# Angle weights before the second chunk, the first angles before the second scores, an early sine, a later wait: retention, token mixer and MLP on one core

## The chip, the cores and the metric

The kernel runs on one core of a Trainium2 chip. The time is device microseconds of one execution, as a median of several. Engines are named as the profile names them: PE is TensorE (PEld its weight loads), DVE is VectorE, ACT is ScalarE, POOL is GpSimd, SP is SyncE; a trailing q, as in SPq, is an engine's sequencer, which also issues DMAs.

## What is computed

Three layers in float32, on 2 batches, 768 tokens and 512 channels (8 heads of 64):

```python
# 1. retention, per head: decayed state, scaled readout
for t in range(S):
    state = gamma * state + outer(k[t], v[t])
    y[t] = scale * (q[t] @ state)
# 2. angles, token mixer, channel layer (x = y with the heads side by side)
theta = x @ w_theta
u = x + w_tok_r @ (x * cos(theta)) + w_tok_i @ (x * sin(theta))
x = u + relu(u @ w_ch)
# 3. MLPs over tokens and over channels
u = x + (relu(x.T @ w_tok1) @ w_tok2).T
out = u + relu(u @ w_ch1) @ w_ch2
```

## The kernel before, in words

**Products.** Most products are done as three reduced-precision matmuls on split operands (helper `three`, L778): each operand is a high part (rounded, written by ACT) plus a low part (the rest, written by DVE or POOL). So every weight and every activation is split before PE can use it. Semaphores order everything; each engine runs its own instruction list strictly in the order written.

**Head of the kernel.** The tokens go through in 12 chunks of 128, numbered g (6 per batch). For a chunk PE runs `scores(g)` (keys times queries, L788), `keys_values(g)` (the chunk's part of the state, L802), `outputs(g)` (L817: first the part read from the state, L827, then the part from the weighed scores, L837), `turn_x` (a transpose, L843) and `theta(g)` (the angles, L854: 12 matmuls that accumulate over 4 channel blocks; for g = 0 the first six wait for the first half of the split angle weights, the other six for the second half). DVE runs `weigh(g)` (L592, scores times the causal decay; it needs `scores(g)`, and `outputs(g)` and `scores(g + 1)` need it), `advance_state` (L597), `finish_x` (L609, it needs `outputs`), `x_low` (L616), and for g = 0 the two `theta_low` (L575), the low halves of the angle weights. ACT runs `x_high` (L473) and for g = 0 the two `theta_high` (L457), later the sine and the cosine of the angles (`waves`, L488). POOL runs `decay_keys(g)` (L377, needs chunk g in memory; it is written one chunk ahead) and `carry_state` (L388).

**Loads.** SP issues in this order: queries and keys of chunk 0 (0.5 MB), its other half (0.5 MB), the output decay (0.25 MB), chunk 1 (1 MB), the two halves of the angle weights (0.5 MB each, into `raw`), chunk 2, a third of a token weight, and then one chunk and one third at a time. Chunk 3 and later wait until `outputs` of the chunk three before has freed the buffer. ACT issues the small constants.

**Order of PE at the start (L882 to L905).** Two dummy matmul calls on a zeroed tile (`keep_warm`), `scores(0)`, `outputs(0)`, `keys_values(0)`, `scores(1)`, `keys_values(1)`, `outputs(1)`, `theta(0)`, `scores(2)`, `keys_values(2)`, `outputs(2)`, `scores(3)`, `turn_x(0)`, `theta(1)`, and from there one such round per chunk.

**Order of DVE at the start (L689 to L714).** `weigh(0)`, `advance_state(0)`, `finish_x(0)`, `weigh(1)`, `x_low(0)`, `theta_low` twice, `advance_state(1)`, `finish_x(1)`, `weigh(2)`, `x_low(1)`, and so on.

**The token mixer** is a two-by-two block scheme of 7 products of 4 steps each (28 steps, `mix`, L865). DVE adds each result into `res` (`keep_y`, L663; semaphore `y_kept`). The last two products write PSUM banks 0 to 3. ACT and POOL split `res` into `ut` (`ut_high`, `ut_low`) for the next layer, the first token half while the mixer still runs.

**The channel layer** (`channels(q)`, L906, 16 steps) writes banks 4 and 5 in turn. Its first step waits for all 28 `y_kept`. `turn_x2(n)` (L921) writes banks 6, 7 and 0 and comes after several channel steps. The MLPs follow.

Of the kernel before, what the change touches and what calls it, by code (L numbers as in the profile page):

```python
# [7 lines left out]
ACT = mybir.ActivationFunctionType  # L8

P = 128  # L10
# [3 lines left out]
NG = B * NC  # L14
# [42 lines left out]
STEPS = PRODUCTS * NPAIR  # L57
# [33 lines left out]
def retention_mixer_mlp(nc, qkv, theta_w, tok, weights, consts, out):  # L91
    with ExitStack() as ctx:
        def sb(name, shape, dt=F32, within=ctx):
            return within.enter_context(nc.sbuf_tensor(name, shape, dt))

        def sem(name):
            return ctx.enter_context(nc.semaphore(name))

        cst = sb("cst", [P, N_CONST])

        res = sb("res", [P, B, NK, S])

# [5 lines left out]
        with ExitStack() as first:  # L108
            idle = sb("idle", [P, DM], within=first)
# [59 lines left out]
        def f32(ap):  # L169
            return ap.bitcast(F32)  # L170
# [23 lines left out]
        def turned(n):  # L194

            return n // 3 % B, n // 6 * 3 + n % 3
# [4 lines left out]
        def tokens(tile, k):  # L201

            return res[:, tile, k, 0:DM] if tile < B else res[:, :, k, DM:S]
# [33 lines left out]
        idle_ready = sem("idle_ready")  # L237
# [25 lines left out]
        y_kept = sem("y_kept")  # L263
# [20 lines left out]
        def split_done(eng, i):  # L284
            if i < MIDDLE:
                eng.wait_ge(middle_lo, i + 1)
            else:
                eng.wait_ge(late_lo, i - MIDDLE + 1)
# [35 lines left out]
        @block.sync  # L324
        def _(sp):
            def load_chunk(g):
                if g >= NQ:
                    sp.wait_ge(y_ready, g - NQ + 1)
                if g == NQ:
                    sp.wait_ge(kv_ready, 1)  # L330
                sp.dma_start(qkv_in[:, g % NQ, :], qkv[g]).then_inc(chunk_in[g % NQ], 16)

            def load_piece(i):
                if i >= NSTAGE:
                    split_done(sp, i - NSTAGE)
                sp.dma_start(stage[:, i % NSTAGE, :], weights[i]).then_inc(piece_in[i % NSTAGE], 16)

            def load_third(e):

                q, at = (2, 1, 0)[1 + e // 3], slice(e % 3 * THIRD, (e % 3 + 1) * THIRD)  # L340
                if e == 3:
                    sp.wait_ge(theta_lo, 2)
                sp.dma_start(raw[:, q, at], tok[2 * q, :, at]).then_inc(third_in[e], 16)

            sp.dma_start(qkv_in[:, 0, 0:2 * DM], qkv[0, :, 0:2 * DM]).then_inc(first_qk_in, 16)
            sp.dma_start(qkv_in[:, 0, 2 * DM:4 * DM], qkv[0, :, 2 * DM:4 * DM]).then_inc(chunk_in[0], 16)
            sp.dma_start(cst[:, C_OUT:N_CONST], consts[:, C_OUT:N_CONST]).then_inc(decay_in, 16)
            load_chunk(1)
            for i in range(2):
                at = slice(i * THETA_HALF, (i + 1) * THETA_HALF)  # L350
                sp.dma_start(raw[:, 0, at], theta_w[:, at]).then_inc(theta_in[i], 16)
            for g in range(2, NG):
                load_chunk(g)
                if g < 8:
                    load_third(g - 2)

            sp.wait_ge(zr_ready, NG)
            sp.wait_ge(zi_ready, NG)
            for i in range(N_PIECES):
                load_piece(i)  # L360
            for tile in range(TILES):
                for n in range(NK):
                    sp.wait_ge(sum_kept, tile * NK + n + 1)
                    to = out[tile, n, :, 0:DM] if tile < B else out[:, n, :, DM:S].rearrange("b p t -> p b t")
                    sp.dma_start(to, tokens(tile, n)).then_inc(out_sent, 16)
            sp.wait_ge(out_sent, 16 * TILES * NK)
# [89 lines left out]
        def _(act):  # L456
# [52 lines left out]
                act.activation(u_half(0, b, k, half), res_half(b, k, half), ACT.Copy).then_inc(ut_hi, 1)  # L509

            act.dma_start(cst[:, 0:C_OUT], consts[:, 0:C_OUT]).then_inc(const_in, 16)
            act.wait_ge(const_in, 16)
            for g in range(NG + 2):
                if g < NG:
# [59 lines left out]
        def _(dve):  # L574
            def theta_low(i):  # L575
                at = slice(i * THETA_HALF, (i + 1) * THETA_HALF)
                dve.wait_ge(theta_hi, i + 1)
                dve.scalar_tensor_tensor(out=w_sq[:, 1, at], in0=raw[:, 0, at], scalar=TURNS, in1=f32(w_sq[:, 0, at]),  # L578
                                         op0=ALU.mult, op1=ALU.subtract).then_inc(theta_lo, 1)
# [12 lines left out]
            def weigh(g):  # L592
                dve.wait_ge(score_ready, g + 1)
                dve.tensor_tensor(prob[:, :, :], ps[:, BK_SCORE:BK_SCORE + 2, :], causal[:, :, :],  # L594
                                  ALU.mult).then_inc(prob_ready, 1)

            def advance_state(g):  # L597
                b, c = g // NC, g % NC
                if c == NC - 1:
                    return  # L600
                dve.wait_ge(kv_ready, b * (NC - 1) + c + 1)
                new, kv = state[:, (g + 1) % 2, :], ps[:, BK_STATE, 0:H * D // 2]
                if c == 0:
                    dve.tensor_scalar(new, kv, 1.0, None, ALU.mult).then_inc(state_ready, 1)
                else:
                    dve.wait_ge(carried_ready, b * (NC - 2) + c)
                    dve.tensor_tensor(new, kv, carried[:, :], ALU.add).then_inc(state_ready, 1)
# [13 lines left out]
            def reduce_angle(g):  # L621
                t = turn[:, g % 2, :]
                dve.wait_ge(whole_ready, g + 1)
                if g >= 2:
                    dve.wait_ge(zi_ready, g - 1)

                dve.scalar_tensor_tensor(out=t, in0=fold[:, g % 2, :], scalar=-ROUND, in1=bank(BK_THETA + g % 2),
                                         op0=ALU.add, op1=ALU.subtract).then_inc(frac_ready, 1)
                dve.wait_ge(frac_ready, g + 1)
                dve.tensor_scalar(t, t, 0.5, -0.5, ALU.min, ALU.max).then_inc(angle_ready, 1)  # L630
# [65 lines left out]
            for g in range(NG + 2):  # L696
                if 0 <= g - 2:
                    reduce_angle(g - 2)
                if g < NG:
                    advance_state(g)  # L700
                    finish_x(g)
                if g + 1 < NG:
                    weigh(g + 1)
                if g < NG:
                    x_low(g)
                if g == 0:
                    for i in range(2):
                        theta_low(i)
                if g >= NG - 1:
                    z_low(g - (NG - 1))  # L710
                if g >= 2:
                    turn_parts(g - 2)
                    if g < 8:
                        token_low(1 - (g - 2) // 3, (g - 2) % 3)  # L714
# [62 lines left out]
        def _(pe):  # L777
# [107 lines left out]
            for g in range(NG):  # L885
                if g and g % NC < NC - 1:
                    keys_values(g)
                outputs(g)
                if g == 0:
                    keys_values(0)  # L890
                if g == 1:
                    theta(0)
                if g + 1 < NG:
                    scores(g + 1)
                if g >= 2:
                    turn_x(g - 2)
                    theta(g - 1)
# [8 lines left out]
            def channels(q):  # L906
                half, b, n = q // (B * NK), q // NK % B, q % NK
                if q == 0:
                    split_done(pe, P_T12 - 1)
                    pe.wait_ge(y_kept, STEPS)  # L910
                if q >= 2:
                    pe.wait_ge(x2_kept, q - 1)
                for k in range(NK):
                    if n == 0:
                        pe.wait_ge(ut_lo, half * B * NK + b * NK + k + 1)
                    mm = three(ps[:, BK_M + q % 2, 0:HS],
                               lambda l: w_sq[:, l, k * DM + n * P:k * DM + (n + 1) * P],
                               lambda r: u_half(r, b, k, half), k == 0, k == NK - 1)
                mm.then_inc(m_ready, 1)

            def turn_x2(n):  # L921
                b, c = turned(n)
                pe.wait_ge(x2_kept, (n // 3 + 1) * NK)
                if n >= 3:
                    pe.wait_ge(x2_lo, n - 2)
                for k in range(NK):
                    mm = pe.transpose(ps[:, BK_X2[n % 3], k * P:(k + 1) * P],  # L927
                                      res[:, b, k, c * P:(c + 1) * P], ident)
                mm.then_inc(x2_ready, 1)
# [141 lines left out]
```

## Time and profile before

| | |
|---|---|
| median of 3 runs | 449.81 us (449.34 to 450.46) |
| profiled execution | 449.38 us, span 447.6 us |
| PE busy | 437.8 us, 98% of the span |
| DVE, ACT, POOL busy | 210.4, 127.9, 99.1 us |
| moved by DMA | 38.29 MB, mean 86 GB/s |

The span runs from the first to the last instruction; the rest of the execution's time lies around it. Busy time says how long an engine worked, not that it set the time. The chain of waits is followed back from the last instruction to whatever released each step. What sets the time at a place is read from that chain and from the idle time in front of an instruction.

### The profile page before, as it was taken

How to read it: one execution, taken by the hardware profiler on the slowest of the kernel's cores; microseconds unless marked ns; L12 is line 12 of the kernel's file. 1: busy time of each engine (PE TensorE's matmuls, PEld its weight loads, DVE VectorE, ACT ScalarE, POOL GpSimd, SP SyncE). 2: the span in 40 equal slices, each digit the busy share in tenths (PEclk: the TensorE clock that was granted, in tenths of full speed). 3: DMA queues.
4: the chain of work that ended last, by engine and by line, in shares of the span. 5: the costliest groups of instructions: out<-in, count | busy, mean ns of one | idle time of the engine just before them, and what ended most of it. 6: DMA issues, size and time to landing. Idle time of an engine off the chain costs nothing.

```text
span 447.6 us, 6232 instructions
## 1 busy us (share of the span) xinstructions
PE 437.8 (98%) x2676; PEld 382.3 (85%) x2676; DVE 210.4 (47%) x304; ACT 127.9 (29%) x194; POOL 99.1 (22%) x80
## 2 busy tenths in 40 slices
PE   7799999999999999999999999999999999999996
PEld 4587878899999999999889888888888888888885
DVE  3789998799999993244335211112211113111113
ACT  0455654734455456012313211111111110111110
POOL 2422241000200009940998940000000000000000
PEclk9999999999999999999999999999999999999999
DMA  8955697540784111030241000000200001000002
GB/s 309 395 218 202 267 235 168 105 142 0 183 182 154 47 49 48 13 129 1 94 142 47 1 0 1 0 0 12 84 1 0 0 1 73 21 1 0 1 0 94
DMA packets 9980, 38.29 MB, mean 86 GB/s; under 512 B 993, under 2 KB 2145, under 8 KB 8161
## 3 DMA queue, kind: packets, MB, share of 16 engines
q1 hardware_dynamic: 7856, 28.31, 17.3%
q0 software_dynamic: 1952, 9.44, 9.2%
q8 instruction: 21, 0.34, 0.3%
q10 hardware_dynamic: 144, 0.14, 0.1%
q14 instruction: 7, 0.05, 0.0%
HBM read 34.75 MB, written 3.15 MB: 85 GB/s over the span
## 4 chain that ended last, share of the span: by engine, by line
PE 95%; DVE 2%; DMA 1%; ACT 1%; issue 0%; DVEq 0%; ACTq 0%
PE ps L780 85%; PE ps L797 3%; PE ps L837 3%; PE ps L851 2%; PE ps L927 1%; PE ps L811 1%; PE ps L827 1%; DMA qkv_in<-qkv 1%; DVE w_sq L578 1%; DVE res L774 1%; DVE prob L594 1%; ACT L477 0%; ACT w_sq L460 0%; ACT x_hi L477 0%; DVE res L613 0%
## 5 line engine op out<-in xcount | busy, mean ns | idle before, releaser
L780 PE MATMUL ps<-u,w_a 128*128 128x512 f32 x432 | 103.3, 389 | 0.0
L768 DVE SCALAR_TENSOR_TENSOR w_sq<-ps,w_sq 128x512 fp32r<-128x512 f32 x36 | 24.9, 692 | 156.7 <-ACT w_sq L561 156.7
L780 PEld LDWEIGHTS ps<-u,w_a 128*128 128x128 f32 x432 | 81.1, 188 | 16.8
L780 PE MATMUL ps<-tw,zs 128*128 128x384 f32 x504 | 88.1, 334 | 0.0
L780 PEld LDWEIGHTS ps<-tw,zs 128*128 128x128 f32 x504 | 87.3, 188 | 0.1
L561 ACT ACTIVATE w_sq<-ps 128x512 fp32r<-128x512 f32 x36 | 21.6, 599 | 168.0 <-PE ps L780 168.0
L780 PE MATMUL ps<-w_sq,ch_a 128*128 128x512 f32 x216 | 51.9, 389 | 0.0
L780 PE MATMUL ps<-w_sq,w_b 128*128 128x512 f32 x216 | 51.4, 389 | 0.0
L780 PEld LDWEIGHTS ps<-w_sq,w_b 128*128 128x128 f32 x216 | 40.5, 188 | 8.4
L780 PEld LDWEIGHTS ps<-w_sq,ch_a 128*128 128x128 f32 x216 | 40.5, 188 | 8.4
L780 PE MATMUL ps<-ut,w_sq 128*128 128x384 f32 x192 | 35.6, 339 | 0.7 <-issue 0.7
L504 ACT ACTIVATE zs<-z 128x768 fp32r<-128x768 f32 x28 | 23.7, 846 | 37.0 <-PE ps L780 37.0
L780 PEld LDWEIGHTS ps<-ut,w_sq 128*128 128x128 f32 x192 | 32.9, 188 | 1.0 <-issue 1.0
L780 PE MATMUL ps<-w_sq,x_hi 128*128 128x512 f32 x96 | 30.8, 402 | 2.3 <-DVE w_sq L578 2.3
L400 POOL TENSOR_TENSOR ut<-res,ut 128x384 fp32r<-128x384 f32 x16 | 16.6, 1068 | 33.0 <-ACT ut L509 33.0
L780 PEld LDWEIGHTS ps<-w_sq,x_hi 128*128 128x128 f32 x96 | 17.1, 188 | 5.9 <-issue 2.2
L584 DVE TENSOR_TENSOR tw<-raw,tw 128x768 fp32r<-128x768 f32 x21 | 20.8, 988 | 0.0
L780 PE MATMUL ps<-w_sq,x_lo 128*128 128x512 f32 x48 | 18.8, 392 | 0.0
L385 POOL TENSOR_TENSOR k_dec<-qkv_in,cst 128x512 f32<-128x512 f32 x10 | 11.5, 1148 | 30.7 <-DMA qkv_in<-qkv 26.8
L731 DVE SCALAR_TENSOR_TENSOR res<-ps,res 128x384 f32<-128x384 f32 x16 | 8.9, 558 | 19.3 <-PE ps L780 19.3
L467 ACT ACTIVATE tw<-raw 128x768 fp32r<-128x768 f32 x21 | 17.4, 830 | 1.0 <-DMA raw<-tok 1.0
L780 PE MATMUL ps<-u,w_b 128*128 128x512 f32 x72 | 17.4, 395 | 0.0
(83 smaller groups left out, 473.1 us busy)
## 6 DMA issues: line engine op xcount, KB each, us to landing
qkv_in<-qkv SPq DMA_DIRECT2D x11, 1024.0 KB, 6.1
stage<-weights SPq DMA_DIRECT2D x17, 512.0 KB, 3.3
raw<-tok POOLq DMA_DIRECT2D x7, 1152.0 KB, 8.9
cols_out<-res SPq DMA_DIRECT2D x12, 256.0 KB, 2.1
raw<-tok SPq DMA_DIRECT2D x6, 384.0 KB, 8.1
raw<-tok POOLq DMA_DIRECT2D x3, 384.0 KB, 9.2
qkv_in<-qkv SPq DMA_DIRECT2D x2, 512.0 KB, 5.0
raw<-theta_w SPq DMA_DIRECT2D x2, 512.0 KB, 8.6
```

The lines of the kernel that those rows point to most:

```text
L385: pool.tensor_tensor(heads(k_dec[:, n % 2, :]), heads(qkv_in[:, g % NQ, 2 * DM:3 * DM]), key_decay, ALU.mult).then_inc(key_ready, 1)
L400: pool.tensor_tensor(u_half(1, b, k, half), res_half(b, k, half), f32(u_half(0, b, k, half)), ALU.subtract).then_inc(ut_lo, 1)
L467: act.activation(tw[:, p % 2, 0, at], raw[:, W_RAW[p], at], ACT.Copy).then_inc(tok_hi, 1)
L504: act.activation(zs[:, s % NZ, 0, :], z[:, Z_KIND[p], i, :], ACT.Copy, scale=Z_SIGN[p]).then_inc(z_hi, 1)
L561: act.activation(h2[:, f % 2, 0, :], bank(BK_H2 + f % 4), ACT.Relu).then_inc(h2_hi, 1)
L584: dve.tensor_tensor(tw[:, p % 2, 1, at], raw[:, W_RAW[p], at], f32(tw[:, p % 2, 0, at]), ALU.subtract).then_inc(tok_lo, 1)
L731: dve.scalar_tensor_tensor(out=part, in0=ps[:, BK_M + q % 2, 0:HS], scalar=0.0, in1=part, op0=ALU.max, op1=ALU.add).then_inc(x2_kept, 1)
L768: dve.scalar_tensor_tensor(out=h2[:, f % 2, 1, :], in0=bank(BK_H2 + f % 4), scalar=0.0, in1=f32(h2[:, f % 2, 0, :]), op0=ALU.max, op1=ALU. ...
L780: mm = pe.matmul(dst, left(l), right(r), start=first and n == 0, stop=last and n == 2, skip_group_check=True)
L797: mm = pe.matmul(ps[:, BK_SCORE + r, i * P:(i + 1) * P], qkv_in[rows, g % NQ, DM + i * P:DM + (i + 1) * P], qkv_in[rows, g % NQ, i * P:(i ...
L837: mm = pe.matmul(ps[cols, BK_Y + r, i // 2 * P:(i // 2 + 1) * P], qkv_in[:, g % NQ, 3 * DM + h * D:3 * DM + (h + 1) * D], prob[:, r, i * P ...
L851: mm = pe.transpose(ps[:, BK_XROW, k * P:(k + 1) * P], res[:, b, k, c * P:(c + 1) * P], ident)
```

## The change

The two loads of the angle weights move ahead of the load of chunk 1. PE runs `theta(0)` right after `keys_values(0)`, ahead of `scores(1)`. DVE runs `weigh(1)` after `x_low(0)` and the two `theta_low`. ACT gets one extra sine of one column at its start, ahead of its wait for the constants; it reads the zeroed tile and nothing reads its result. In the channel layer the wait for all 28 `y_kept` moves from the first channel step to the first `turn_x2`.

```diff
@@ sync @@
-            load_chunk(1)
             for i in range(2):
                 at = slice(i * THETA_HALF, (i + 1) * THETA_HALF)
                 sp.dma_start(raw[:, 0, at], theta_w[:, at]).then_inc(theta_in[i], 16)
+            load_chunk(1)
@@ scalar @@
             act.dma_start(cst[:, 0:C_OUT], consts[:, 0:C_OUT]).then_inc(const_in, 16)
+
+            act.wait_ge(idle_ready, 1)
+            act.activation(spare[:, :], idle[:, 0:1], ACT.Sin)
             act.wait_ge(const_in, 16)
@@ vector @@
-                if g + 1 < NG:
+                if 0 < g < NG - 1:
                     weigh(g + 1)
                 if g < NG:
                     x_low(g)
                 if g == 0:
                     for i in range(2):
                         theta_low(i)
+                    weigh(1)
@@ tensor @@
                 outputs(g)
                 if g == 0:
                     keys_values(0)
-                if g == 1:
                     theta(0)
                 if g + 1 < NG:
                     scores(g + 1)
@@ channels @@
                 if q == 0:
                     split_done(pe, P_T12 - 1)
-                    pe.wait_ge(y_kept, STEPS)
@@ turn_x2 @@
                 pe.wait_ge(x2_kept, (n // 3 + 1) * NK)
+                if n == 0:
+                    pe.wait_ge(y_kept, STEPS)
```

## Rows read from the trace of the kernel before

**Rows 1.** The page: busy time, share and instructions of each engine; the granted clock.

```profile
PE 437.8 (98%) x2676; PEld 382.3 (85%) x2676; DVE 210.4 (47%) x304; ACT 127.9 (29%) x194; POOL 99.1 (22%) x80
...
PEclk9999999999999999999999999999999999999999
```

**Rows 2.** Chain that ended last, in order of time: start us, us, what.

```profile
5.36 2.10 PE ps L797 x16
...
9.94 0.49 PE ps L811 x16
...
10.95 0.61 DVE res L613
...
11.63 1.28 ACT L477
...
12.92 0.63 ACT x_hi L477
13.55 0.96 ACT w_sq L460
...
17.80 1.65 PE ps L780 x6
19.45 1.12 PE ps L797 x16
...
20.59 1.24 DVE prob L594
...
21.87 1.09 PE ps L837 x16
...
24.64 2.75 PE ps L780 x12
27.40 0.62 PE ps L811 x16
28.01 0.60 PE ps L827 x16
```

**Rows 3.** Timeline of PE at the first angles: start us, us, line, [idle before <-releaser].

```profile
15.91 0.70 PE L780 MATMUL ps<-w_sq,x_hi 128*128 128x512 f32 x2 [1.99 <-DVE w_sq L578]
```

**Rows 4.** Timeline of DVE and POOL around the split of the angle weights.

```profile
14.53 1.23 DVE L578 SCALAR_TENSOR_TENSOR w_sq<-raw,w_sq 128x1024 fp32r<-128x1024 f32 x1 [0.26 <-ACT w_sq L460]
...
15.68 2.07 DVE L578 SCALAR_TENSOR_TENSOR w_sq<-raw,w_sq 128x1024 fp32r<-128x1024 f32 x1
...
9.81 1.04 POOL L385 TENSOR_TENSOR k_dec<-qkv_in,cst 128x512 f32<-128x512 f32 x1 [2.05 <-DMA qkv_in<-qkv]
14.86 1.80 POOL L385 TENSOR_TENSOR k_dec<-qkv_in,cst 128x512 f32<-128x512 f32 x1 [4.01 <-DMA qkv_in<-qkv]
```

**Rows 5.** Timeline of SP, then the last line of the view of L351.

```profile
2.81 0.97 SPq L351 DMA_DIRECT2D raw<-theta_w  x2
...
DMA to landing us min/median/max: 8.2/8.6/9.0
```

**Rows 6.** Groups by line: every table load of ACT.

```profile
L477 ACT ACT_TABLE_LOAD x1 | 1.3, 1283 | 11.6 <-DVE res L613 11.6
L494 ACT ACT_TABLE_LOAD x1 | 1.3, 1283 | 0.0
```

**Rows 7.** Timeline of PE's first work; scores (L797) at 6.3 us, then chunks 0 to 3.

```profile
1.46 3.78 PE L786 MATMUL ps<-idle 128*128 128x512 f32 x4 [1.46 <-DVE idle L689]
...
L797 PE MATMUL ps<-qkv_in x6: 417/418/418, 6.0 to 6.4; 64*128 64x128 f32 x6
...
L797 PE MATMUL ps<-qkv_in x64: 272/272/579, 5.4 to 23.8; 64*128 64x128 f32 x64
```

**Rows 8.** Timeline, 170 to 180 us: the end of the mixer, the channel layer's start.

```profile
168.46 11.74 POOL L400 TENSOR_TENSOR ut<-res,ut 128x384 fp32r<-128x384 f32 x11 [33.02 <-ACT ut L509]
...
175.47 0.56 DVE L687 TENSOR_TENSOR res<-res,ps 128x384 f32<-128x384 f32 x1 [2.57 <-PE ps L780]
...
176.13 4.05 PE L780 MATMUL ps<-ut,w_sq 128*128 128x384 f32 x22 [0.69 <-issue]
```

More of the change, by code:

```diff
@@ L99, in retention_mixer_mlp @@
         cst = sb("cst", [P, N_CONST])
+        spare = sb("spare", [P, 1])
         res = sb("res", [P, B, NK, S])
```

## The prediction

> **What bounds the kernel now.** I read the page first. PE is busy for 98% of the span and nothing else comes near [rows 1], so an edit can pay or cost only where PE stands still or where the order of its work changes. The chain of waits says where: from 21.87 us on it holds PE alone, apart from one hole of 0.69 us at the channel layer (below) and the last additions into the result. Before 21.87 us it hops between engines [rows 2]. So I worked out the head of the kernel step by step up to `outputs(2)`, which starts its second part at 21.87 us, and took the rest as PE work that shifts with it. The rounds that follow cannot soak up a shift, since each engine's list there is unchanged and PE never waits.
>
> In the head the reader is to see two chains. One leads to the angles: `finish_x(0)` ends at 10.95 + 0.61 = 11.56, a table load of 1.28, `x_high` 0.63, the first `theta_high` 0.96, then `theta_low` twice on DVE, and PE's last six angle matmuls 17.80 + 1.65 = 19.45 [rows 2]. PE waits for it: 1.99 us ahead of the first angle matmul [rows 3], while it has already done `scores(1)` and `outputs(1)` in the time before. The other is the loop scores, `weigh`, `outputs`: scores 1.12, `weigh` 1.24, small gaps; from 19.45 to 21.87 that is 2.42 us, during which PE has `keys_values` and the state part of `outputs` (0.62 + 0.60) to do beside `weigh` [rows 2].
>
> **The table load.** The extra sine puts a table load near 1.5 us, where ACT has nothing to do until 11.56. Will the later ones go? The trace has two: one before the first copy, one before the first sine, and none after it, though copies, absolute values and ReLUs follow [rows 6]. So the set that holds the sine holds the rest, and both loads go from their places. The second was on ACT alone. The first is in the chain: 1.28 us. `x_high(0)` then runs 11.63 to 12.26, the first `theta_high` to 13.22, and `theta_low` could start at 13.24 instead of 14.53. The Trainium skill (ScalarE: Activation LUTs, What ACT_TABLE_LOAD costs) gives about 2.7 us for a load; the row says 1.28. By the page the gain would be 1.4 us more.
>
> **The loads.** The second half of the angle weights was issued at about 3.3 us and took 9.0, so it landed at 12.3; the first landed at 2.81 + 8.2 = 11.0 [rows 5]. ACT would want them at 12.26 and 13.22. Earlier loads therefore gain nothing by themselves. But chunk 1 trades places with them: the same bytes stand ahead of it as stood ahead of the second half, so it lands near 12.3. Behind it is `decay_keys(1)` on POOL, which ran at 9.81 and took 1.04 [rows 4]; now it starts at about 12.3 to 13.0, in the middle of DVE's splitting.
>
> **What POOL then costs.** The trace shows such a meeting. `decay_keys(2)` started at 14.86, when chunk 2 landed, and took 1.80 instead of 1.04, with the first `theta_low` (14.53 to 15.76, 1.23 us) beside it; the second `theta_low` took 2.07 instead of 1.23 [rows 4]. The extra times fit an order of turns: POOL waits for the first, the second waits for POOL; the second ended 17.75 - 15.76 = 1.99 after the first. After the change there are two such meetings. `x_low(0)` and `decay_keys(1)` end at about 14.0 together (12.3 + 0.69 + 1.04, in either order, give or take 0.1). The first `theta_low` goes from 14.0 to 15.2. `decay_keys(2)` still comes at 14.86 (the bytes ahead of chunk 2 are the same), so the second `theta_low` ends at 15.2 + 1.99 = 17.2. PE's second six follow: 17.25 + 1.65 = 18.9. Of the 1.28 us of the table load only 19.45 - 18.9 = 0.55 is left.
>
> **The order of PE.** Before, `scores(1)`, `weigh(1)` and `outputs(1)` ran in the shadow of the angle chain. Now they stand behind `theta(0)`, and nothing of PE's can fill the shadow: from 9.94 + 0.49 = 10.43 to about 15.3 PE is idle. After the angles come scores and `weigh` (2.42), the second part of `outputs(1)` (1.09), and again scores and `weigh` (2.42): 5.93 us, so that `outputs(2)` starts its second part at 18.9 + 5.93 = 24.8 instead of 21.87. Head: +2.9 us. `keys_values(1)` and the state part of `outputs(1)` stay beside `weigh(1)`, at a gap of 0.1 at most. `weigh(1)` moved on DVE delays nobody: DVE is free at 17.2 and the scores come at 20.0. Chunk 4 waits for `outputs(1)` and is issued 8 us later (near 22 instead of 13.96), but `scores(4)` is needed only after `theta(1)`, beyond 28.01 + 2.9, and 9 us from issue to landing is the longest of rows 5; if it came 1 us late, that would add 1 us, which I leave to the range.
>
> **The channel layer.** The last `mix` ends about 175.4; DVE's last `keep_y` runs 175.47 to 176.03; `channels(0)` starts at 176.13 after 0.69 us of idle [rows 8]. Its data is the first token half, all of it split long before: POOL begins that half at 168.46 and needs about 1.07 each for 8, done at 172. Its bank was last read two products earlier. So the hole closes: -0.69 us, at worst 0. Where the wait went, at the first `turn_x2`, it is over some 12 us before PE arrives.
>
> **The sum.** +2.9 - 0.7 = +2.2 to +2.3 us. Against the profiled execution's own 449.38 us (span 447.6) this gives 451.6; that run lies 0.43 below the median of 449.81, so the median to expect is 452.1, +0.5%. About 0.3% is what a measurement of this kernel can tell from no change, so 448.5 to 451.2 counts as the same.
>
> **Rival 1: PE's clock falls in the new pause.** The granted clock in the page reads 9 in every slice [rows 1], yet the durations show two levels: a score matmul takes 418 ns at 6.3 us and 272 ns later, and the 16 of `scores(0)` took 2.10 us against 1.12 [rows 2, 7], so PE ran at 1.2 GHz for its first 5.6 us of work (from 1.46 to past 7.0) and then at 2.4 GHz. The pauses that it withstood here are at most 2 us; the new one is 4.9. If PE comes back at the lower level for as long as at the start, until about 20.9, the first six angle matmuls (2.75 / 2 warm) take 2.8 and end at 18.1, the second six take 3.3 in place of 1.65, and end at 21.4 instead of 18.9: +2.5, and part of the next scores up to +1.0. With +3.0 the median is 455.1. For it: the pause is more than twice any that the trace has. Against it: no row shows a fall after work has begun. If it comes but lifts again by 18 us, it costs only 0.2 and my forecast stands. The Trainium skill (TensorE: Matmul & The Clock Gate, HAM oscillation) warns that pauses between bursts of matmuls bring the half-rate clock back; by it this rival would be the forecast. Chance 0.27.
>
> **Rival 2, on the other side: POOL and DVE do not meet.** If chunk 1 lands so early that `decay_keys(1)` is over by 12.3 (landing before 11.2), the first `theta_low` starts at 13.24. Without the second meeting either, both end at 13.24 + 2 x 1.23 = 15.7, the angles at 17.4, `outputs(2)` at 23.3: head +1.45, sum +0.8, 450.6, no measurable change. With the second meeting alone: 13.24 + 3.22 (as from 14.53 to 17.75) + 1.70 = 18.2, sum +1.5, 451.4. It decides for "the same" once the angles end before 18.0. Against it: the queue's order. Chance 0.18. To be faster by over 0.3% the angles would have to end before 15.3, which two `theta_low` alone rule out on these rows; I keep 0.05 for what they don't show.
>
> **Rival 3: the edits don't do what they say.** The table load stays in its place (+1.3) or the hole at the channel layer stays (+0.7): 452.8 to 453.4. Against it rows 6 and 8. Chance 0.05.
>
> **How the numbers follow.** The forecast has 0.45: 452.1, its own range 451.3 to 453.0. Faster 0.05, same 0.18, slower 0.77 (0.45 + 0.27 + 0.05). The range goes from Rival 2's 450.6 to Rival 1's 455.2; it leaves out the faster case and the worst of the clock case.
>
> **What would show each step.** One table load, near 1.5 us, and `x_high(0)` at 11.6. `decay_keys(1)` near 12.3 to 13, and one or both of `x_low(0)` and it longer than 0.69 and 1.04. `theta_low` near 14.0 and ending near 17.2. PE idle for about 4.9 us before the first angle matmul; those matmuls at about 390 ns (clock kept) or near double. `outputs(2)`'s second part at 24.8. No idle ahead of `channels(0)`. The prediction is wrong if the second part of `outputs(2)` starts within 0.7 us of 21.87, or if PE has new idle time beyond it.

## The result and the profile after

| | before | changed |
|---|---|---|
| median, 7 runs each | 450.27 us (449.34 to 450.65) | 452.72 us (451.63 to 453.44) |
| ratio | | 1.0054, 95% interval 1.0038 to 1.0071 |
| profiled execution | 449.38 us, span 447.6 | 452.98 us, span 451.2 |

The change costs 2.45 us, or 0.54%. A second set of runs of the changed kernel gave 1.0061 (1.0037 to 1.0085). The two profiled executions lie 3.6 us apart, more than the medians: before's was 0.9 us quicker than its median and the changed one's 0.3 us slower. Sums from the traces have to be made against the 3.6. One of the twelve executions of the experiment e8 below took 2505 us, which no trace explains; its ratio leaves that one out.

The page after, the busy times and the granted clock (lines 1 and 2, to be held against [rows 1]):

```profile
PE 440.0 (98%) x2676; PEld 384.4 (85%) x2676; DVE 211.3 (47%) x304; ACT 127.3 (28%) x194; POOL 98.4 (22%) x80
...
PEclk9699999999999999999999999999999999999999
```

PE has the same 2676 instructions and is busy 2.2 us longer: its work itself got slower. The 6 in the second slice says where. The chain that ended last, in order of time (start us, us, what; [rows 2] is its counterpart; ... marks what is left out, mostly gaps under 0.15 us):

```profile
12.30 1.46 DVE x_lo L622
13.76 1.15 DVE w_sq L582
...
15.05 5.46 PE ps L785 x12
20.51 1.42 PE ps L802 x16
...
21.95 1.24 DVE prob L598
...
23.23 1.09 PE ps L842 x16
24.33 1.12 PE ps L802 x16
...
25.47 1.24 DVE prob L598
...
26.75 1.09 PE ps L842 x16
...
29.52 2.73 PE ps L785 x12
```

The table load is gone from the chain. The twelve angle matmuls take 5.46 us in one piece, where `theta(1)` takes 2.73. Then scores, `weigh`, `outputs` run twice, one after the other, and `outputs(2)` starts its second part at 26.75 instead of 21.87. The same twelve by stretches of time (start and end, length, then the busy time of PE, PEld, DVE, ACT and POOL); the column before the last two is PE's granted clock as a share of 2.4 GHz:

```profile
12.00:14.00 2.00, 0.00 (x0) 0.00 (x0) 1.70 (x2) 2.00 (x3) 1.04 (x1) 1.00 0.95 402
14.00:16.00 2.00, 0.95 (x2) 0.83 (x3) 2.00 (x2) 0.16 (x1) 1.33 (x2) 0.57 1.08 446
16.00:18.00 2.00, 2.00 (x6) 1.57 (x5) 0.88 (x1) 0.00 (x0) 1.35 (x1) 0.50 0.94 392
18.00:20.00 2.00, 2.00 (x6) 1.40 (x5) 0.00 (x0) 0.00 (x0) 0.00 (x0) 0.50 0.13 51
20.00:22.00 2.00, 2.00 (x23) 1.44 (x23) 0.05 (x1) 0.00 (x0) 0.00 (x0) 0.72 0.03 8
```

PE did nothing from 10.4 us on, the clock fell to 1.2 GHz at about 14.3, inside the pause, and came back at about 21.1. The table load, the splitting of the angle weights, and POOL beside it, from the timeline (start us, us; [rows 3, 4, 6] before):

```profile
1.16 1.28 ACT L515 ACT_TABLE_LOAD   x1 [1.16 <-PEq L1069]
...
12.17 1.04 POOL L386 TENSOR_TENSOR k_dec<-qkv_in,cst 128x512 f32<-128x512 f32 x1 [4.47 <-DMA qkv_in<-qkv]
...
12.30 1.46 DVE L622 TENSOR_TENSOR x_lo<-res,x_hi 128x512 fp32r<-128x512 f32 x1 [0.76 <-ACT x_hi L478]
13.69 3.19 DVE L582 SCALAR_TENSOR_TENSOR w_sq<-raw,w_sq 128x1024 fp32r<-128x1024 f32 x2
14.67 1.13 POOL L386 TENSOR_TENSOR k_dec<-qkv_in,cst 128x512 f32<-128x512 f32 x1 [1.46 <-DMA qkv_in<-qkv]
...
15.05 1.19 PE L785 MATMUL ps<-w_sq,x_hi 128*128 128x512 f32 x2 [4.65 <-DVE w_sq L582]
```

`decay_keys(1)` came with chunk 1 at 12.17, and `x_low(0)`, 0.69 us long when alone, took 1.46. And the start of the channel layer ([rows 8] before):

```profile
180.15 4.15 PE L785 MATMUL ps<-ut,w_sq 128*128 128x384 f32 x23
180.35 0.55 DVE L691 TENSOR_TENSOR res<-res,ps 128x384 f32<-128x384 f32 x1 [2.56 <-PE ps L785]
```

PE is in the channel layer before DVE's last `keep_y` has begun, with no idle time.

### The profile page after: what moved, and what is told of

Its sections match the earlier page's. It is cut to its first block, busy times and chain, and to the rows that moved or that the text cites. A ratio compares the mean times of both kernels' runs of the same rounds, so it can differ in the third digit from the quotient of the medians.

```text
span 451.2 us, 6233 instructions
## 1 busy us (share of the span) xinstructions
PE 440.0 (98%) x2676; PEld 384.4 (85%) x2676; DVE 211.3 (47%) x304; ACT 127.3 (28%) x194; POOL 98.4 (22%) x80
## 4 chain that ended last, share of the span: by engine, by line
PE 96%; DVE 2%; DMA 1%; issue 0%; ACT 0%; DVEq 0%; ACTq 0%
PE ps L785 85%; PE ps L802 3%; PE ps L842 3%; PE ps L856 1%; PE ps L932 1%; PE ps L816 1%; PE ps L832 1%; DMA qkv_in<-qkv 1%; DVE prob L598 1%; DVE res L779 1%; DVE x_lo L622 0%; DVE w_sq L582 0%; ACT x_hi L478 0%; DVE res L617 0%; DVE state L608 0%
## 5 line engine op out<-in xcount | busy, mean ns | idle before, releaser
L785 PE MATMUL ps<-w_sq,x_hi 128*128 128x512 f32 x96 | 32.5, 421 | 4.6 <-DVE w_sq L582 4.6
L785 PEld LDWEIGHTS ps<-w_sq,x_hi 128*128 128x128 f32 x96 | 18.3, 200 | 8.2 <-issue 4.8
L478 ACT ACTIVATE x_hi<-res 128x512 fp32r<-128x512 f32 x12 | 7.6, 632 | 43.8 <-DVE res L617 43.8
L785 PE MATMUL ps<-w_sq,x_lo 128*128 128x512 f32 x48 | 19.8, 412 | 0.0
L598 DVE TENSOR_TENSOR prob<-ps,causal 128x1024 f32<-128x1024 f32 x12 | 14.6, 1220 | 8.0 <-PE ps L802 8.0
```

Of the source, the lines that this page charges most:

```text
L478: act.activation(x_hi[:, g % 2, :, :], res[:, g // NC, :, g % NC * P:(g % NC + 1) * P], ACT.Copy).then_inc(x_hi_ready, 1)
L785: mm = pe.matmul(dst, left(l), right(r), start=first and n == 0, stop=last and n == 2, skip_group_check=True)
```

## The experiments

Every run is compared with the kernel before on the same chip. Ratios are comparable across all runs; medians less so, since the kernel before itself stood at 449.5 to 450.3 us. Its single times ranged from 447.9 to 451.9, which matters below. "Head" is the time from the start of `outputs(0)` to the start of the second part of `outputs(2)` in the profiled execution, which leaves out how early `outputs(0)` began. It is one execution of each kernel, and the later chunks land at their own times, so it varies too: 17.91 and 17.69 for the changed kernel, 12.67 with a fall of the clock and 11.19 without one for e4 and e12, which are the same kernel. For every execution the mean granted clock over its whole span is on record as well. e4's profiled execution, at the lower level again from 7.7 to 11.2 us, reads 0.996; the changed kernel's, from 14.3 to 21.1, reads 0.992; one without a fall reads 0.999 or 1.000.

| kernel | ratio to before (95%) | median us | head us |
|---|---|---|---|
| before | 1 | 449.5 to 450.3 | 13.02 |
| changed | 1.0054 (1.0038 to 1.0071) | 452.72 | 17.91 |
| e5: changed, again | 1.0061 (1.0037 to 1.0085) | 452.08 | 17.69 |
| e1: changed + dummies | 1.0012 (0.9990 to 1.0033) | 450.18 | 15.57 |
| e2: before + wait | 0.9972 (0.9949 to 0.9995) | 448.81 | 12.48 |
| e3: before + sine | 0.9940 (0.9917 to 0.9963) | 447.02 | 11.29 |
| e4: before + sine + wait | 0.9934 (0.9910 to 0.9957) | 446.81 | 12.67 |
| e12: the same again | 0.9920 (0.9896 to 0.9943) | 446.11 | 11.19 |
| e7: e4 + loads | 1.0006 (0.9990 to 1.0023) | 449.64 | 14.44 |
| e6: e4 + order | 1.0054 (1.0038 to 1.0071) | 451.84 | 17.41 |
| e8: e6 + dummies | 1.0005 (0.9988 to 1.0023) | 449.72 | 14.72 |
| e11: before + order | 1.0109 (1.0081 to 1.0136) | 454.52 | 18.25 |
| e9: e4 + dummy in first pause | 0.9911 (0.9886 to 0.9935) | 445.90 | 11.20 |
| e10: before + the same dummy | 0.9980 (0.9962 to 0.9997) | 449.13 | 13.03 |

**The clock.** e1 fills PE's pause with dummy matmuls on the zeroed tile.

```diff
                     keys_values(0)
+                    keep_warm(4, DM)
                     theta(0)
```

> The changed kernel with four dummy matmul calls (128x512, on the zeroed tile, the same as at the start) put ahead of theta(0), so that PE works through most of the pause from 10.4 to 15.05 us. If the fall of the clock to half in that pause costs what the trace of the changed kernel suggests, the angle matmuls go back to about 390 ns, theta(0) ends near 18.6 instead of 20.5, outputs(2) starts its second part near 24.5 instead of 26.75, and the time falls by 2 to 2.3 us against the changed kernel: 450.4 to 450.7, within 0.1% of the kernel before. If the clock is a bystander (the angle chain and the order of PE cost all of it), the time stays at 452.7. If the dummies themselves are late, theta(0) starts after 15.3.

Measured: 1.0012 instead of 1.0054, about 2 us less. Stretches of e1, with the granted clock as above:

```profile
14.00:16.00 2.00, 1.37 (x6) 1.19 (x7) 1.62 (x2) 0.00 (x0) 1.13 (x1) 1.00 1.07 443
16.00:18.00 2.00, 2.00 (x16) 1.45 (x16) 0.00 (x0) 0.00 (x0) 1.09 (x2) 1.00 0.95 395
```

The clock stays at its upper level. The head shrinks from 17.91 to 15.57, 2.34 us. PE did four calls more of work and the kernel became faster: e1's twelve times lie between 449.8 and 451.0, the changed kernel's thirteen between 451.6 and 453.4. So the cost of the lost clock is shown, not argued.

**The two parts that pay.** e2 moves only the wait, e3 adds only the sine, e4 does both; e12 is e4 again.

> The kernel before with only the wait for y_kept moved. My sum says -0.7 us; the trace of the changed kernel says -0.9 (mixer plus channel layer took 0.94 us less, since the first weight load is pulled ahead too). Nothing at all if DVE's last keep_y is late for something else. 449.3 to 449.6 against 450.27.

> The kernel before with only the early sine. The plain sum: -1.28 us. My reading of the turns between POOL and DVE says more: x_high(0) at 11.6, x_low(0) at 12.8 after weigh(1), theta_low at about 13.5 and 14.7, so the second one is issued ahead of decay_keys(2) at 14.86 and is not held off (1.23 instead of 2.07 us); theta(0) ends near 17.6 instead of 19.45, outputs(2) starts its second part near 20.0 instead of 21.87, -1.9 us: 448.4. If turns do not matter, 449.0. If another wait takes the place of the load, no change.

> Early sine and moved wait, with the loads and the orders of PE and DVE as before. If the two parts add, -1.9 - 0.9 = -2.8 us, 447.5, 0.6% faster than before. Then the loads and the order carry the whole loss of the change: 452.7 - 447.5 = 5.2 us.

> Sine and moved wait alone once more, as the yardstick beside the run with the dummy in the first pause: 446.8, in two groups near 445.9 and 446.9.

e2 measured -1.0 to -1.3 us (0.9972), with a wide interval; the expected -0.7 to -0.9 is inside it. In the profiled executions e2 is 1.32 us ahead of the kernel before at the second part of `outputs(2)` (20.55 against 21.87), where nothing was edited, and 2.27 ahead at the last additions (439.74 against 442.01): the moved wait itself gives 0.95. e3 measured 0.9940, -2.7 us, more than the 1.9 of its own reading and twice the plain 1.28; the head went from 13.02 to 11.29, -1.73. Its timeline:

```profile
12.22 0.68 DVE L622 TENSOR_TENSOR x_lo<-res,x_hi 128x512 fp32r<-128x512 f32 x1
...
12.82 2.35 DVE L582 SCALAR_TENSOR_TENSOR w_sq<-raw,w_sq 128x1024 fp32r<-128x1024 f32 x2
...
15.22 1.05 POOL L386 TENSOR_TENSOR k_dec<-qkv_in,cst 128x512 f32<-128x512 f32 x1 [4.28 <-DMA qkv_in<-qkv]
```

Both `theta_low` are done before chunk 2 brings `decay_keys(2)`: 2.35 us for the pair, against 3.22 where POOL came between them [rows 4]. Taking 1.28 us out of the chain also took DVE out of POOL's way. e12 shows it from the same start as the kernel before (`outputs(0)` at 8.86 against 8.85): the pair took 2.36 us and the head 11.19. The sine is not the only way out of the meeting. In e2, where `outputs(0)` began 0.78 us sooner and the table load was in the chain, the pair took no longer:

```profile
13.76 2.36 DVE L578 SCALAR_TENSOR_TENSOR w_sq<-raw,w_sq 128x1024 fp32r<-128x1024 f32 x2 [0.25 <-ACT w_sq L460]
```

So some executions of the kernel before pay for the meeting and others need not. Of the 2.6 us between the spans of e3 and of before (445.0, 447.6), 1.73 is the head, 0.53 is that `outputs(0)` began sooner (8.32 against 8.85), and 0.3 lies behind the start of the last additions (439.74 against 442.01, 2.27 apart). e3's twelve times lay within 446.8 and 447.3, where those of the kernel before spread over 4 us.

In the median e4 gave hardly more than e3 (0.9934 and 0.9920 against 0.9940), but the medians mix executions with and without a fall of the clock. All twelve of e3 read a mean clock of 0.999 or 1.000, only four of e4's ten did. Without a fall e3 took 446.8 to 447.3, e4 and e12 445.7 to 446.3: the moved wait adds about 1.0 us to the sine, as it did alone. Why e3 had no fall and e4 six is open.

**Loads and order.** e7 is e4 with the angle weights loaded first, e6 is e4 with the new orders of PE and DVE, and the changed kernel has both, so the four make a square. The edits are the first, third and fourth hunks of the diff.

> The changed kernel itself, as the yardstick beside the next three. 452.7 us, the ratio to the kernel before near 1.0054 to 1.0065. If the fall of the clock is a matter of chance from run to run, its times stand in two groups about 2 us apart.

> The changed kernel with chunk 1 loaded ahead of the angle weights again; sine, wait and both orders as changed. decay_keys(1) goes back to 9.8 us and meets neither x_low(0) nor theta_low. If that meeting is what held the angle chain: x_low(0) 0.69 us long, theta_low from 13.24, its second one at 14.5 ahead of decay_keys(2), both done at 15.7 instead of 16.9. PE's pause is then 4.2 instead of 4.6 us. If the clock falls as in the changed kernel, PE is the bound of the angles and only their earlier start counts: -0.45 us, 452.2. If the shorter pause keeps the clock, the angles end at 17.35: -3.2 us, 449.5. If POOL was a bystander, no change.

> Sine and moved wait with the angle weights loaded first, but both orders (PE and DVE) as before: the load order alone. scores(1) has to wait for chunk 1 until 12.2 instead of 9.9 us; weigh(1) follows at 13.3 and holds back x_low(0) to 14.5 and theta_low to 15.2 or, when decay_keys(2) gets in first, 16.2. theta(0) ends at 19.5 to 20.4 against 17.1 in the run with the early sine alone: +2.4 to +3.3 on 446.8, so 449.2 to 450.1. If the load order is harmless, 446.8.

Measured on the base of e4 and e12 (0.9934, 0.9920): loads +0.7 to +0.9%, order +1.2 to +1.3%, both +1.2 to +1.4%. The loads cost about 3 us where `scores(1)` runs early, since PE then waits for chunk 1, and `weigh(1)`, `x_low(0)` and `theta_low` all come after it: the first angle matmul starts 8.91 us after `outputs(0)` (17.41 - 8.50) against 5.80 in e12, and e7's median of 449.64 is within the expected 449.2 to 450.1. From e7's waits (who waited for what, us in total, times, longest):

```profile
PE ps L801 <- DMA qkv_in<-qkv: 2.2, 1, 2.2
```

Where `theta(0)` runs first they cost next to nothing. e6 shows what they do there: with chunk 1 first, `x_low(0)` was 0.69 us long again, the two `theta_low` took 2.36 together, and the first angle matmul came 5.78 us after `outputs(0)` began instead of 6.21 (14.27 - 8.49 against 15.05 - 8.84), the expected -0.45. e6's timeline:

```profile
11.95 0.69 DVE L622 TENSOR_TENSOR x_lo<-res,x_hi 128x512 fp32r<-128x512 f32 x1 [0.76 <-ACT x_hi L478]
...
12.89 2.36 DVE L582 SCALAR_TENSOR_TENSOR w_sq<-raw,w_sq 128x1024 fp32r<-128x1024 f32 x2 [0.25 <-ACT w_sq L461]
```

At the lower clock PE bounds the angles, so that start is all that is gained. The clock fell in e6 as well, although its pause was 4.2 us instead of 4.6. The thirteen times of the changed kernel lie between 451.6 and 453.4, with no group 2 us lower, and twelve of them read a mean clock of 0.989 to 0.992, so the fall comes in nearly every execution, not by chance. The thirteenth read 0.999 and was no quicker, 453.37 us; it has no trace, and its cause is open.

**The order by itself.** e8 is e6 with e1's dummies: neither the meeting with POOL nor the fall of the clock. e11 is the kernel before with the new orders alone.

> As e6_chunk1_first with the four dummy calls ahead of theta(0) as in e1_after_warm: neither the meeting with decay_keys(1) nor the fall of the clock. What is left against the run with sine and wait alone is the order of PE. theta(0) ends at 17.35, outputs(2) starts its second part at 23.3 against about 20.0 there: +3.3 on 446.8, so 450.1 by the chain; by e1_after_warm (450.2, whose outputs(2) started 1.1 later) 449.1. If the order of PE cost nothing, 446.8.

> The kernel before with the new orders of PE and DVE alone: table load in the chain, chunk 1 first, old wait. The pause of PE is then 10.4 to 15.9, 5.5 us. With the clock kept the angles end at 19.45 as before and outputs(2) starts its second part 3.5 us later (5.93 - 2.42): 453.1. With the fall, which the pause of 4.6 us brought in the changed kernel, the twelve angle matmuls take 5.46 us from 15.9 on, +1.9 more: 455.0. If the order of PE were harmless, 449.6.

e8's head is 14.72 against e12's 11.19: 3.53 us, and the two `weigh` loops of the prediction's sum say 5.93 - 2.42 = 3.51. The angles start equally long after `outputs(0)` in both (5.78 and 5.80 us), so nothing but the order is left between them. `outputs(0)` and the second part of `outputs(2)` in e8, then in e12:

```profile
8.75 1.09 PE L842 MATMUL ps<-prob,qkv_in 128*64 128x128 f32 x16 [1.41 <-DVE prob L598]
...
23.47 1.09 PE L842 MATMUL ps<-prob,qkv_in 128*64 128x128 f32 x16
```

```profile
8.86 1.09 PE L841 MATMUL ps<-prob,qkv_in 128*64 128x128 f32 x16 [1.41 <-DVE prob L598]
...
20.05 1.09 PE L841 MATMUL ps<-prob,qkv_in 128*64 128x128 f32 x16
```

In the ratios it is 0.7 to 0.85%, 3.2 to 3.8 us; e8's median, 449.72, lies between the two that were expected. e8 against e1 would show the meeting with `decay_keys(1)` at the full clock: 0.85 us in the head, but 1.0005 against 1.0012 in the times, which is inconclusive. e11 is the worst kernel of all, +4.9 us by its ratio and 454.52 in the median (455.0 was expected with the fall), with the twelve angle matmuls, nearly all at the lower level, from 15.61 to 20.8. Its timeline where PE's pause ends:

```profile
15.61 1.19 PE L781 MATMUL ps<-w_sq,x_hi 128*128 128x512 f32 x2 [5.51 <-DVE w_sq L578]
```

**Short pauses.** In e4's profiled execution the clock had risen before the first scores, as nowhere else, and PE then waited 1.52 us for `weigh(0)`. The timeline of PE in e4, and below it the stretches of e4 with the granted clock:

```profile
7.91 1.98 PE L841 MATMUL ps<-prob,qkv_in 128*64 128x128 f32 x16 [1.52 <-DVE prob L598]
```

```profile
6.00:8.00 2.00, 0.48 (x10) 0.29 (x8) 1.82 (x2) 0.00 (x0) 1.04 (x1) 0.93 1.07 441
8.00:9.00 1.00, 1.00 (x10) 1.00 (x12) 0.00 (x0) 0.00 (x0) 0.00 (x0) 0.50 0.98 414
```

The clock fell in that pause, and `outputs(0)` took 1.98 us instead of 1.09. e9 and e10 put a dummy there.

```diff
             scores(0)
+            keep_warm(1, DM // 2)
```

> Sine and moved wait, loads and orders as before, and one dummy matmul call of 256 columns between scores(0) and outputs(0), where PE waits 1.4 us for weigh(0). In the look at the run with sine and wait the clock had risen before scores(0), fell in just this pause, and outputs(0) took 1.98 us instead of 1.09. If pauses as short as this let the clock fall in some executions, the slower group of that run (446.8 to 447.5) goes and the times stand at 445.8 to 446.0 (median 446.0). If the two groups come from something else, the median stays at 446.8. The dummy cannot delay outputs(0): 0.86 us even at the lower clock, in a pause of 1.4.

> The kernel before with the same dummy call in the same place and nothing else. Its own times range from 447.9 to 451.9. If the fall of the clock in the pause after scores(0) makes part of that spread, the median falls by 0.5 to 1.5 us, to 448.3 to 449.3, and the times above 451 go. If the spread comes from the meeting of POOL and DVE alone, nothing changes: 449.6.

e9 measured 0.9911 and 445.90 us, all its times between 445.7 and 446.2. It beats both kernels, but it overlaps e12. Its times are those of e4 and e12 without a fall (445.7 to 446.3), so the dummy can save a fall and gives nothing else; with four executions, how often it does is not settled. e10 measured 0.9980 (0.9962 to 0.9997): the dummy alone is worth about 0.9 us to the kernel before. The mean clocks say where that comes from. Nine of its twelve executions read 0.999 or 1.000, against four of the 17 of the kernel before on the same chip.

The same record sorts the spread of the kernel before over all 78 executions: the 31 that read 0.999 or 1.000 took 447.9 to 449.6 us, the 34 at 0.994 to 0.996 took 449.4 to 450.7, and the 13 at 0.991 or 0.992 took 451.6 to 451.9. So the slow ones are those that spent longer at the lower clock. In which pause it fell in them is not shown: that e10 had fewer falls speaks for the pause after `scores(0)`, and that three of its executions still read 0.995 or 0.996 speaks for another pause as well.

## Why the prediction was right, and where it was not

The forecast was 452.1 us and +2.3; measured were 452.72 and +2.45. The number is right in part by luck: the cost of the clock, which the sum did not have, was made up for by how far before's profiled execution lay below its median. Against the profiled executions' +3.6 the sum was 1.3 short:

- **Table load: right.** One load, at 1.16 us, and `x_high(0)` at 11.64 (forecast 11.63). The row stays at 1.28 us. The Trainium skill (ScalarE: Activation LUTs, What ACT_TABLE_LOAD costs) gives 1283 ns for the load itself and 1380 ns for a drain, which make up its 2.7 us; the prediction set the whole against the row. The load agrees with the row, the drain does not show: before, the load ahead of the first sine ended at 27.64 and the sine began at 27.66, and the early sine moved `x_high(0)` by 1.28 us (12.92 to 11.64).
- **POOL against DVE: right in kind, 0.3 us too dear.** `decay_keys(1)` at 12.17 (12.3), `theta_low` from 13.76 to 16.88 (14.0 to 17.2). The Trainium skill (SBUF — State Buffer, Who interferes with whom) has a DVE instruction with two inputs in SBUF contend with a GpSimd one that reads SBUF, and the order of issue decide which of them is held up; the trace agrees: `x_low(0)`, issued 0.13 us after `decay_keys(1)`, took 1.46 us for 0.69. In e5, the same kernel, `x_low(0)` began sooner and `decay_keys(1)` met the first `theta_low` instead; the angles started as late (6.29 us after `outputs(0)`, here 6.21). e6 and e3 show both meetings gone when their cause is.
- **Order of PE: right.** 3.51 us by the sum, 3.53 between e8 and e12. At the full clock the head grew by 15.57 - 13.02 = 2.55 us, where the sum had 2.9.
- **Channel layer: 0.3 us too small.** In the chains the shift goes from +4.88 (29.52 against 24.64 [rows 2]) to +3.89 at the last additions (445.90 against 442.01). I had counted only the 0.69 of idle. e2, with the wait alone, gives 0.95 as well, so it belongs to the wait. Part of the other 0.3 fits the first weight load: it starts 0.17 us ahead of the first matmul in e2 (173.77, 173.94) and in the changed kernel, and 0.03 ahead before (176.10, 176.13).
- **The clock: the step that failed.** Rival 1, at a chance of 0.27, is what happened, and in every run with a long pause ahead of `theta(0)` and no dummies. It cost 2.3 us in the head (17.91 - 15.57), not 3.0. The low level ended at about 21.1, near the 20.9 that I had assumed, but the angles ended at 20.51 and not at 21.4: the second six took 2.76 us, where I had doubled 1.65 to 3.3 although six take only half of `theta(1)`'s 2.73 at the upper level, and the first six began at 15.05 and took 2.70. Of `scores(1)` only 0.3 us was caught (1.42 for 1.12). The rival's median is 455.1 by the prediction's own sum; the 455.2 in its range is a slip. I read "no row shows a fall after work has begun" as evidence against it. One execution that stood two short pauses said nothing on a pause of twice their length; e4 shows a fall in 1.5 us. The warning of the Trainium skill (TensorE: Matmul & The Clock Gate, HAM oscillation) should have made it the forecast.

What separates the sum's +2.3 from the profiles' +3.6 is: -0.4 for the head at the full clock, -0.3 for the channel layer, -0.3 at the very end (the last additions are 3.9 us later but the span only 3.6 longer), +2.3 for the clock, together +1.3. The medians differ by only 2.45 because before's median was 0.9 us above its profiled execution, for which I had put 0.43, and the changed kernel's 0.3 below its own. Before's profiled execution read a mean clock of 1.000, while 47 of its 78 others on record read 0.996 or less: the typical execution of the kernel before pays something for the clock too.

The last additions in the chain, of the kernel before and then of the changed one:

```profile
442.01 2.73 DVE res L774 x4
```

```profile
445.90 2.73 DVE res L779 x4
```

The second table load of the kernel before and the sine behind it:

```profile
26.36 1.28 ACT L494 ACT_TABLE_LOAD   x1
27.66 0.72 ACT L494 ACTIVATE fold<-fold,cst 128x512 f32<-128x512 f32 x1
```

Rival 2 did not come true: chunk 1 landed where the queue's order put it. Rival 3 neither. Chunk 4, left to the range, cost nothing: from 26.75 us on the chain holds PE alone up to the last additions.

## What to carry to other kernels

Moving a consumer ahead on an in-order engine takes away the work that filled its wait: here two chains that had run side by side came to stand in a row, and the early loads did nothing to pay for that. Ask of each new pause of TensorE whether it can keep the clock, and price the work behind it at both levels; a few dummy matmuls in the pause settle the question in one run. Of a bundle of edits, run each alone: two of these four were worth 0.7 to 0.8% together, and the other two lost all of it and 0.5% more.

## What the runs showed of the hardware

The clock first rose at different moments in executions of like kernels: the 16 first scores took 2.10 us before, 1.32 in e2 and 1.16 in e4, and `outputs(0)` began at 7.91 to 8.86 us. It then fell in a pause of 1.5 us in e4, where one of 1.4 kept it in the other profiled executions, and in e7 near 13.4 us, after a wait of 2.2 us for chunk 1 and with PE at work again since 12.25 (stretches of e7):

```profile
12.00:14.00 2.00, 1.75 (x28) 1.60 (x30) 0.55 (x1) 1.83 (x2) 1.04 (x1) 0.86 0.95 403
14.00:16.00 2.00, 2.00 (x32) 1.55 (x30) 2.00 (x3) 0.00 (x0) 1.24 (x1) 0.50 1.06 441
```

The low level that the kernel starts with reads 1.00 in the granted clock: the scores at 6.3 us ran at 418 ns beside a full column [rows 1, 7]. Only durations show that one, and so a mean of 1.000 does not say that the first rise came early.
